# Chunks of 64-token units, pipelined over their borders, in the first MLP of an attention and two-MLP kernel

## The reference

```
# _attn_ref, for each batch and head
q_d, k_d, v_d = mean of q, k, v over groups of 4 rows         # 144 rows
out_up   = repeat(softmax(q_d k_d^T / 8) v_d, 4)              # pooled attention, each row 4 times
out_local = softmax(q k^T / 8 masked to |i - j| < 4) v        # band of 7 offsets
x = tokens x (heads*64) of (out_up + out_local)
# _moe_ref:  h = x @ w_in (512 x 2048);  x2 = max(h, 0)^2 @ w_out (2048 x 512)
# _moe2_ref: h = max(x2 @ w1, x2 @ w2, x2 @ w3) (512 x 768); out = h @ w_out (768 x 512)
```

## Time and profile before

| | |
|---|---|
| median of 3 runs | 931.53 us |
| profiled execution: span from first to last instruction | 929.1 us |
| TensorE (PE) busy | 828.0 us (89%) |
| VectorE (DVE) busy | 582.4 us (63%) |
| ScalarE (ACT) busy | 341.3 us (37%) |
| GpSimd (POOL) busy | 245.8 us (26%) |
| moved by DMA | 47.68 MB, 51 GB/s over the span |

### The profile page before, as it was taken

How to read it: one execution, slowest core, us unless ns; L and a number is a source line. 1 busy time by engine, 2 the same in 40 slices (tenths; PEclk the granted TensorE clock), 3 DMA queues, 4 the chain that set the end, 5 groups by cost and what they waited for, 6 DMA issues and landing times.

```text
span 929.1 us, 13196 instructions
## 1 busy us (share of the span) xinstructions
PE 828.0 (89%) x5292; PEld 777.6 (84%) x5292; DVE 582.4 (63%) x655; ACT 341.3 (37%) x897; POOL 245.8 (26%) x213
## 2 busy tenths in 40 slices
PE   0545878899997899997999999999999999999995
PEld 0333878789997789996889999999999999999994
DVE  6888999877999876999777983752222221212211
ACT  1543443745433745343645444331121212121111
POOL 4166894212444213353214343210000000000000
PEclk9999989999999999999999999999999999999998
DMA  8232353100124100224100002632020111100001
GB/s 191 59 102 68 87 135 85 52 2 1 52 60 97 40 1 1 61 50 111 26 2 1 26 1 77 190 93 68 1 68 1 35 35 35 35 28 8 12 23 34
DMA packets 41293, 47.68 MB, mean 51 GB/s; under 512 B 6928, under 2 KB 33424, under 8 KB 40336
## 3 DMA queue, kind: packets, MB, share of 16 engines
q1 hardware_dynamic: 41232, 46.83, 18.6%
HBM read 36.21 MB, written 10.62 MB: 50 GB/s over the span
## 4 chain that ended last, share of the span: by engine, by line
PE 63%; DVE 26%; ACT 4%; POOL 2%; issue 2%; DMA 1%; SPq 0%; ACTq 0%; DVEq 0%
PE PS L368 19%; PE PS L370 18%; PE PS L369 18%; DVE tmp L792 4%; DVE sc L793 4%; DVE qb L820 4%; DVE pooled L698 3%; DVE tmp L819 3%; DVE x L884 3%; PE PS L394 2%; ACT qkT L563 2%; PE PS L410 2%; POOL W L954 2%; PE PS L375 1%; PE PS L401 1%
## 5 line engine op out<-in xcount | busy, mean ns | idle before, releaser
L368 PE MATMUL PS<-XS,W 128*128 128x288 f32 (+1 forms) x912 | 292.5, 321 | 0.8 <-POOL W L954 0.8
L369 PE MATMUL PS<-XS,W 128*128 128x288 f32 (+1 forms) x912 | 288.2, 316 | 0.0
L370 PE MATMUL PS<-XS,W 128*128 128x288 f32 (+1 forms) x912 | 288.1, 316 | 0.0
L981 POOL TENSOR_TENSOR G<-g,G 128x288 fp32r<-128x288 f32 x128 | 141.2, 1103 | 269.4 <-ACT G L605 269.4
L368 PEld LDWEIGHTS PS<-XS,W 128*128 128x128 f32 x912 | 173.8, 191 | 2.8 <-POOL W L954 1.0
L369 PEld LDWEIGHTS PS<-XS,W 128*128 128x128 f32 x912 | 173.5, 190 | 1.5
L370 PEld LDWEIGHTS PS<-XS,W 128*128 128x128 f32 x912 | 173.3, 190 | 0.0
L368 PE MATMUL PS<-G,W 128*128 128x288 f32 x512 | 159.1, 311 | 10.6 <-POOL G L981 10.6
L369 PE MATMUL PS<-G,W 128*128 128x288 f32 x512 | 152.5, 298 | 0.0
L370 PE MATMUL PS<-G,W 128*128 128x288 f32 x512 | 152.1, 297 | 0.0
L920 DVE TENSOR_TENSOR t<-PS,t 128x384 f32<-128x384 f32 x36 | 20.1, 557 | 156.5 <-PE PS L370 156.4
(11 more groups left out here) (90 smaller groups left out, 1064.1 us busy)
## 6 DMA issues: line engine op xcount, KB each, us to landing
qb<-q SPq DMA_DIRECT2D x8, 576.0 KB, 5.7
vb<-v SPq DMA_DIRECT2D x4, 1152.0 KB, 7.8
XR<-x_scratch SPq DMA_DIRECT2D x6, 768.0 KB, 4.9
out<-osb SPq DMA_DIRECT2D x36, 128.0 KB
WR<-moe_w_out SPq DMA_DIRECT2D x15, 256.0 KB, 2.6
kb<-k SPq DMA_DIRECT2D x3, 1152.0 KB, 8.1
WR<-moe_w SPq DMA_DIRECT2D x12, 256.0 KB, 3.2
WR<-moe_w_in SPq DMA_DIRECT2D x11, 256.0 KB, 2.8
```

The source lines that it names most:

```text
L368: mm(dst, wt(HI), xt_(HI), start=first, stop=False)
L369: mm(dst, wt(HI), xt_(LO), start=False, stop=False)
L370: return mm(dst, wt(LO), xt_(HI), start=False, stop=last)
L981: Q.tensor_tensor(G[:, f % NGR, LO, :cnt], g32[:, f % 2, :cnt], G[:, f % NGR, HI, :cnt].bitcast(f32), ALU.subtract).then_inc(g_ready, 1)
```

## The change

**Chunks.** Token order is by units of 64 tokens (4 rows of each of the 16 groups). The first MLP has 9 chunks of 2, 3, 4 units (batch 0) and 5, 4 units (batches 1 to 3): 128, 192, 256, and 320 and 256 tokens. One loop over all 144 steps replaces the loop per chunk, so `up` of a chunk's first steps comes between the last two `down` of the one before. `read_x2` (copying the accumulators out) comes after the square of step 1 instead of before step 0. `XS` holds two chunks.

```diff
-    PLACES = ((0, 18), (18, GL))
+    U = POOL * NG
+    CU = [0, 2, 5, 9]
+    for b in range(1, NB):
+        CU += [NJ * b + 5, NJ * b + NJ]
+    NCH = len(CU) - 1
+    CNT = [U * (CU[n + 1] - CU[n]) for n in range(NCH)]
...
+            for s in range(TOTAL + LAG):
+                if s < TOTAL:
+                    up(s)
+                if s == TOTAL - 1:
+                    up2(0)
+                for b, task in PLAN.get((s, 0), []):
+                    attend(b, task)
+                if s >= LAG:
+                    down(s - LAG)
+                for b, task in PLAN.get((s, 1), []):
+                    attend(b, task)
```

```diff
+                        if w == 2:
+                            last = nc.tensor.transpose(ps[:, at], view(pqk[:, j], "p w d -> p (w d)"), ident[:])
+                        else:
+                            for r in range(POOL):
+                                i = POOL * j + r
+                                last = mm(ps[:D, at], k_rows(i, i + 1)[:, 0] if w else qk[:, i, :],
+                                          ident[:], start=r == 0, stop=r == POOL - 1, is_transpose=True)
```

```diff
+                    pe.wait_ge(band_out, n + 1)
+                    for m in range(2 * (j1 - j0)):
+                        i = POOL * j0 + 2 * m
+                        last = nc.tensor.transpose(ps[:, P * m:P * (m + 1)], view(qk[:, i:i + 2, :], "p r d -> p (r d)"), ident[:])
...
+                    for r in range(2):
+                        for e in range(2):
+                            src = view(ps[64 * r:64 * r + 64, :4 * cnt], "p (m g c e) -> p e c m g", g=NG, c=KC, e=2)[:, e]
+                            dst = view(x32[64 * e:64 * e + 64, :, :cnt], "p c (m r g) -> p r c m g", r=2, g=NG)[:, r]
+                            last = A(dst, src, ACT.Copy)
```

```diff
+            def scale_pooled(b):
+                read(dve, b, ("o", NH - 1))
+                link(V.tensor_scalar(rec[:], view(hst[:, 1], "p h n -> p (h n)"), EPS, float(POOL), ALU.add, ALU.mult))
+                link(V.reciprocal(rec[:], rec[:]))
+                o = view(od_st, "p (c d) -> p c d", d=D)
+                V.tensor_tensor(o, o, rec[:].unsqueeze(2).broadcast_to([SB, 2 * NH, D]), ALU.mult).then_inc(od_scaled, 1)
+            def add_pooled(n):
+                b, (lo, hi) = BATCH[n], ROWS[n]
+                dve.wait_ge(od_loaded, 16 * (b + 1))
...
+                V.tensor_tensor(acc, acc, add, ALU.add).then_inc(band_out, 1)
```

**Weights.** Raw weights land where their LO part will be, without a ring: ten loads in groups of 2, 2, 4, 4, 4 steps' columns, issued at once after v. VectorE splits tiles 0 to 3, ScalarE and GpSimd 4 to 17 before chunk 0, the other 14 in its steps 0 to 6, two each. The second MLP's loads land in place too:

```diff
+            def load_w2(f):
+                sp.wait_ge(up_done, TOTAL - NF + 2 * f + 2)
+                sp.wait_ge(down_done, TOTAL - NF + 2 * f + 2)
...
             load_x2(0)
+            for f in range(NF2):
+                load_w2(f)
```

More of the change, by code:

```diff
@@ new lines, in attention_and_two_mlps, with put @@
+    heads0 = []
+    for n in range(NH + 2):
+        heads0 += [("s", n)] if n < NH else []
+        heads0 += [("t", n - 1)] if 1 <= n <= NH else []
+        heads0 += [("o", n - 2)] if n >= 2 else []
+    heads = []
+    for n in range(NH + 3):
+        heads.append(([("o", n - 3)] if n >= 3 else []) + ([("s", n)] if n < NH else []))
+        heads.append([("t", n - 2)] if 2 <= n < NH + 2 else [])
+    first_tasks = qk_tasks(0) + heads0 + X[:1]
+    PLAN = {}
+    def put(n, f, e, b, tasks):
+        PLAN.setdefault((NF * n + f, e), []).extend((b, t) for t in tasks)
@@ L96, in attention_and_two_mlps @@
[L96 to L100, removed]
+        prs = sb("prs", [P, 2 * 4 * SD], f32, c1)
+        ods = sb("ods", [P, 2 * NH * D], f32, c1)
+        odg = sb("odg", [P, NJ, D], f32, c1)
+        x32 = sb("x32", [P, KC, 2 * U], f32, c1)
@@ L158, in x_before @@
[L158 to L180, removed]
-        dups = qk_tasks + xt[0] + xt[1]
-        dup_of = {t: i for i, t in enumerate(dups)}
-        def dup_use(b, task):
-            return b * len(dups) + dup_of[task]
@@ L389, in attend @@
                     if h == 0:
[L390 removed]
+                        for t in qk_tasks(b):
                             read(pe, b, t)
@@ new lines, in split_w, with run, bufs @@
+            def split_w(i):
+                w_landed(dve, i)
+                link(V.tensor_copy(w_tile(i, HI), w_raw(i)))
+                V.tensor_tensor(w_tile(i, LO), w_raw(i), w_tile(i, HI).bitcast(f32), ALU.subtract).then_inc(w_ready_dve, 1)
+            def run(steps_of, count_=BAND):
+                for _ in range(count_):
+                    if next(steps_of, steps_of) is steps_of:
+                        return
+            def bufs(n, all_):
+                cnt = ROWS[n][1] - ROWS[n][0]
+                return [tmp[:, :cnt]] + ([early[:, 0, :cnt], early[:, 1, :cnt]] if all_ else [])
@@ new lines, in _ @@
+            dve.wait_ge(q_loaded[1], 16)
+            dve.wait_ge(k_loaded, 32)
+            seg1 = score_steps(1, bufs(1, True))
+            for h in range(2, NH):
+                head_max(0, h)
+                if h % 2:
+                    run(seg1, 1)
+                elif h // 2 - 1 < W_BY_DVE:
+                    split_w(h // 2 - 1)
+            run(seg1, 1)
+            split_w(W_BY_DVE - 1)
+            scale_pooled(0)
+            run(seg1)
+            softmax_in(1)
+            add_pooled(0)
```

1044 lines of the change are left out of this document (521 added, 523 removed).

## The result

1010.67 us (median of 4 runs, 1009.93 to 1011.63) against 931.66 for the kernel before: ratio 1.0855, 95% interval 1.084 to 1.0871. Forecast were 893 us, range 868 to 925.

The account below looks back on a forecast made before the run. Bounds: TensorE, busy 89%, and at first VectorE, as no MLP runs until 18 rows of attention finish. Start 74, first MLP 408.3+58+31 = 497, second 316.6+3: span 890.6, plus 2.4 outside, 893 us; range 868 to 925.

Parts of the forecast that it names:

- Matmuls: First MLP, nine chunks of 384 matmuls priced in proportion to columns: 408.3 us against 403.5 before, a cost of 4.8.
- rival (a): Chunks 0 and 1: narrow matmuls don't scale but cost the plain f32 price, 2.2 ns a column; whole 1068 us; chance 0.13.
- turning point: Chunks 0 and 1 together: the narrow-matmul rival decides from 38 us more, 0.16 us a matmul.
- The argument against the floor: Stationary-tile load of 107 ns for 128 columns: held not to set a floor, since transposes, loads included, took 0.088 us.
- smaller ones and restarts at the lower clock: First MLP, among the 31 us of stalls that stay: small waits and low-clock restarts, 3 us.
- Chunk 0 paced by GpSimd, 47 us: Chunk 0: GpSimd's late weight splits hold seven steps at 4.1 us, then nine near 2; 47 us against 25, 22 lost.
- Start: Before the MLPs: TensorE waits for 8 rows, not 18; first `up` at 74 us instead of 91.1, bounds 65 to 91.
- Woven work and VectorE from batch 1 on: First MLP: woven attention costs TensorE 58 us, gain 2; VectorE's batch falls to 101.5 us under TensorE's floor of 119.
- TensorE should no longer wait for it: From batch 1 on: TensorE no longer waits for VectorE; before, a batch took 136.5 us against a floor of 123.
- rival (b): Each batch's `head_max`: VectorE stays late, 11 to 13 us a batch remain; whole 918 us; chance 0.2.
- Second MLP: Second MLP: weight loads now wait for the last chunk's steps, cost 3 us (0 to 6); the rest stays 316.6.
- what VectorE sheds: VectorE, per batch: sheds head normalisation, 20 additions into x and some sums; busy falls from 117.1 to 101.5 us.

Follow-up runs that it names:

- m1: Matmuls alone, the whole computation left out: groups of one width at full clock, then after 34 us pauses; 301 of 128 columns take 64.8 us, of 192 36.8.
- m2: Matmuls alone without pauses, each narrow group right behind 512-column ones at full clock; 128 columns over 128 stationary ones cost 0.112 us each.
- e4: The changed kernel with chunk 0's matmuls padded from 128 to 192 columns, chunk 1 as it is; 980.17 us, ratio 1.054 to the kernel before.
- e1: The changed kernel with chunks 0 and 1 padded with zeros to 256 columns; 987.03 us, ratio 1.0605 to the kernel before.
- e3: The changed kernel, batches 1 to 3: last two head maxima between next band's scores; batches 2 and 3: exponential requested before q and k sums; 985.54 us.
- e9: e7 with denser heads in batch 1, x tasks rescheduled, six late splits for ten, q and k summed after the fourth score; 930.61 us, ratio 0.9998.
- e6: The changed kernel with batch 0 in two chunks (256, 320 columns), four more weight tiles split ahead, old k/q order, VectorE order of e3; 940.95 us.
- e11: The changed kernel with 40 unread 512-column matmuls ahead of chunk 0 to raise the clock, chunk 0 still 128 wide; 1005.36 us, ratio 1.0799.
- e10: e9 with the exponential of chunk 1's band back at step 3 of chunk 0, some x tasks one step later; 925.17 us, ratio 0.9934.
- e7: e6 without VectorE's 17.2 us exponential wait, k and v loaded first, batch 1's k transposes in chunk 0, first two maxima before the values; 940.63 us.

## Why the prediction was wrong

- *Matmuls*, the step that failed: "a column costs 0.00042 us", drawn from 288 and 384 columns down to 128 and 192, which made 0.0655 and 0.092 us. What the runs showed instead is a floor set by the 128 stationary columns, 0.112 us at 2.4 GHz and 0.213 at 1.2; in m1 224 moving columns still stand on it, 256 cost 0.120. By it, chunks 0 and 1 cost 384 x 0.213 = 82 and (17 us at the low clock, 80 matmuls, then 304 x 0.112 = 34) 51 us, measured 78.3 and 51.8 with some `down`s of each beyond its border. That is rival (a) by another mechanism than the one priced there; its turning point, 38 us more in the two chunks, was passed with 48.
- The argument against the floor was a misreading. The Trainium skill ("TensorE: Matmul & The Clock Gate", LDWEIGHTS) gives 107 ns for 128 stationary columns; m2 has 0.112 us at full clock, 5% more. The prediction set against it 0.088 us a transpose, the 0.35 us from the first of four woven transposes to the first matmul behind them. But that matmul in turn has 0.21 or 0.22 us to its next, where the others have 0.13. From one group of transposes to the next, in the trace of before:
```profile
558.61 0.60 PE L375 MATMUL PS<-ident,dup 128*128 128x128 f32 x4
558.96 0.38 PE L368 MATMUL PS<-XS,W 128*128 128x288 f32 x1
559.17 0.29 PE L369 MATMUL PS<-XS,W 128*128 128x288 f32 x1
559.30 0.29 PE L370 MATMUL PS<-XS,W 128*128 128x288 f32 x1
...
560.62 0.60 PE L375 MATMUL PS<-ident,dup 128*128 128x128 f32 x4
```
  Between these starts lie four transposes and twelve matmuls of 288 columns: 2.01 us, less 12 x 0.133, leaves 0.105 us a transpose. The row that was read as evidence against the floor stood near it.
- *The clock* had no term beyond "smaller ones and restarts at the lower clock". It is the larger part: e4, whose matmuls stand at the floor with the clock mostly full, needs 98.9 us for chunks 0 and 1, the changed kernel 130.1, the forecast had 82. So at least 31 of the 48 us are the low clock, at most 17 the floor together with GpSimd's pace. At full clock the floor alone would have made chunk 1 43 us for 35, and chunk 0 would have hidden it.
- *Chunk 0 paced by GpSimd, 47 us*: hidden under a TensorE that was slower still. In e1 it shows: 57.1 us, 10 more than booked. There G and two splits take 5 us a step at first (G's LO parts start at 90.92, 95.97 and 101.61), where 4.1 were booked and the matmuls take 3.
- *Start*: 79.9 for 74, within the bounds; TensorE's wait of 9.7 us for pooled v, until 45.0, had not been seen.
- *Woven work and VectorE from batch 1 on*: "TensorE should no longer wait for it" failed. VectorE has time (105.5 us busy in the 138.2 of chunks 3 and 4), and is late all the same: rival (b)'s picture with another cause, an order of waits and not load. e3 brought 25 of the 65.5 us. Of chunk 2's 95 us TensorE is idle 21.7. From the last head's product (276.0) to chunk 3's first `up` (304.67) 28.7 us go by in a row, with TensorE idle for 17 of them: scaling, the trip through DRAM, the addition (until 288.5), then three x tasks, 16 us where the prediction had 8. The first x task's copies start only at 294.57, since ScalarE's program has the exponential of the next band before them, and ScalarE waits 10.8 us for VectorE to have its scores ready:
```profile
294.36 0.30 ACT L594 ACTIVATE sc<-sc 128x112 f32<-128x112 f32 x1 [10.77 <-DVE sc L797]
```
  No run moved that exponential alone, so its price, some 5 us at the most, is read and not shown. e9 starts the heads denser, and chunk 1 there takes 88.5 us with five units where e6 took 104.6.
- *Second MLP* and *what VectorE sheds* came as forecast (317.7; 516.3 us busy for 582.4).
- Not settled: why 128 columns hold a high clock alone (m2) and don't bring it back once it is down (m1, e11). Of the 65.5 us beyond the narrow chunks, only e3's 25 were recovered by an edit to the changed kernel itself; the rest was read from waits and from e6 to e10, which change several things at once. The pairs still take 132.3 and 129.5 us in e3 for 120.5, with TensorE busy 126.1 and 121.9 of them: that remainder was not taken apart.

## What to carry to other kernels

Where each matmul brings a new stationary tile, price narrow moving sides by the stationary columns: no f32r matmul here cost less than 0.112 us over 128 of them. A first chunk cut below the width where the moving side decides (between 224 and 256 columns here) saves nothing a matmul, and zeros as padding can be faster, since the clock may hang on the width. A chunk more is a full sweep over all weight tiles: 384 x 0.112 = 43 us at the least here, for any width. When a woven group is priced from a timeline, measure from one group to the next, so that the lengthened distance behind it is counted. Before an engine's wait is removed, ask who uses the time: GpSimd's splits were fast while VectorE waited, and it was worth 5 us to put that wait back (e10).

## What the runs showed of the hardware

- After 34 us of standstill, f32r matmuls of 128 columns over 128x128 tiles stay at 1.2 GHz for 64.8 us of unbroken work (m1); 192 columns reach 2.4 GHz after 6 us, 128 columns over 64 stationary ones after 4.
- At 2.4 GHz, 128 columns hold it through 45 us without a wait (m2), 64 columns lose it within 5 us. Behind a wait of 1.05 us 128 columns lose it and don't get it back (e11, 78 us); 256 columns lose it behind one of 1.75 us, the third of its kind, and have it back 3.4 us later (e1).
- Price by stationary columns at 2.4 GHz with 128 moving: 128: 0.112 us, 96: 0.085, 64 and 32: 0.060. 64 moving over 128 stationary cost 0.213 us at the low clock, as 128 do (m2, 80 to 135 us).
- A GpSimd subtraction over 128 x 512 takes 1.3 us while VectorE waits and 2.3 to 2.5 beside its products with v (e7, e9, e10).
